# Attention stage of a fused attention and mixing kernel: three engines' loops written out, waits against constants, covered waits left out

## The chip, the cores and the metric

The kernel runs on one core of a Trainium2 chip. The metric is the device time of one execution in microseconds (us). Before the change three runs took 1269.08, 1270.90 and 1271.06 us, median 1270.9.

## What is computed

Inputs are q, k, v of shape (8, 8, 576, 64), batch, heads, sequence, head dimension, in float32, and the weights of two mixing layers.

```python
scores = scale * np.matmul(q, k.transpose(0, 1, 3, 2))
thresh = np.max(scores, axis=-1, keepdims=True) - tau
scores = np.where(scores >= thresh, scores, -1000000000.0)
attn = np.exp(scores - np.max(scores, axis=-1, keepdims=True))
attn = attn / (np.sum(attn, axis=-1, keepdims=True) + 1e-09)
x = np.matmul(attn, v)                  # then heads side by side: (8, 576, 512)
...
xk, xr = mu_k * x + (1 - mu_k) * x_prev, mu_r * x + (1 - mu_r) * x_prev
x = sigmoid(xr @ w_r) * (np.maximum(xk @ w_k, 0.0) ** 2 @ w_v)
gate = sigmoid(causal convolution of x with 5 taps)
out = (gate * (x @ w_val)) @ w_out
```

## The kernel before

Each engine has its own program, and the programs meet in semaphores alone: an instruction raises a count when it is done, and a wait holds an engine until a count is reached. The kernel has two stages. The attention stage takes the 64 heads in 32 pairs. The mixing stage takes the sequence in 16 halves and isn't touched; TensorE's program for it is already written out.

In the attention stage a pair of heads (2 x 576 queries) makes nine score tiles of 128 queries by 576 keys: tiles 0 to 7 alternate between the heads, tile 8 (MIX) holds the last 64 queries of both. For each tile TensorE makes the scores into one of three PSUM slots (`score_ps`, L606; four matmuls of 288 columns, six for tile 8), VectorE takes the row maximum (`max`, L791), ScalarE the exponential (`exp`, L717), and VectorE multiplies it with the mask of the threshold and sums the row (`mask`, L803, followed by a read of the accumulator, which raises `probs_ready`). A `thr` step (L797) makes the thresholds of two tiles at a time. Then TensorE transposes the tile's four blocks (`probs`, L549) into one of two further PSUM banks (`aux_ps`), ScalarE copies the bank out (L697) and raises `aux_copied`, and after all tiles TensorE multiplies with v (`pv0`, `pv1`, L651). The remainders go the same way (`rem0`, `rem1`). The next pair's q and k are transposed by TensorE (`k0`, `q0`, and `kq0`, one block of both remainders), copied by ScalarE, split into a high and a low part by GpSimd, and stacked below one another by DMA from SyncE's queue.

The order on each engine is written out by hand in a plan, and a step with a minus belongs to the pair before:

```python
PE_PLAN = steps("""
    scores1 kq0 scores3 k0 pv0- scores2 probs4- scores4 q0 rem1- scores0 probs5- scores8 probs1
    probs7- scores6 probs6- probs8- scores7 probs3 pv1- rem0 scores5 probs0 probs2
""")
DVE_PLAN = steps("""
    max1 max3 thr4- mask5- thr0 sum0- mask1 mask3 max2 recip0- max4 thr1 mask2 max0 mask4 max8 thr2
    mask0 max6 max7 thr3 mask8 mask6 mask7 max5
""")
```

The number is that of the tile, not of the turn. A score step waits in `probs_ready` for the mask of the tile three turns earlier, which had its slot: scores8 for the mask of tile 2, scores7 for that of tile 0. Steps that write a bank of `aux_ps` wait in `aux_copied` for the copy two groups earlier: kq0 for the copy of probs0.

`walk` (L329) runs the plans: the first pair, then a hardware loop of 15 rounds with two pairs each (pairs 1 to 30), then the last pair without k, q and kq, and a drain. In the loop, the count that a wait needs depends on the round, so it is computed in a register by `count`, `count_later`, `turns`; in the first pair, the last and the drain the round is the number 0 and the counts are constants. GpSimd's and SyncE's programs of this stage have loops of their own. At the end of the stage the drain overlaps with the mixing stage's first matmuls.

Of the kernel before, what the change touches and what calls it, by code (L numbers as in the profile page):

```python
# [14 lines left out]
TILES = 9  # L15
MIX = 8
# [99 lines left out]
def attention(nc, banks, semaphore, q, k, v, tau, small_loads, x_first, weights, x_scratch, recip_scratch, w_hi, w_lo,  # L116
# [18 lines left out]
    with ExitStack() as ctx:  # L135
# [409 lines left out]
        def tensor(pe):  # L545
# [21 lines left out]

            def run(plan, it, c):
                for kind, i, before in plan:
                    cc = c - 1 if before else c  # L570
                    if kind in GROUPS:
                        g = number(c, (kind, i, before))
                        if g >= 2:
                            pe.wait_ge(aux_copied, turns(it, g - 1))
                        bank = aux_ps[g % 2]
                        blocks = bank[:].rearrange("p (t q) -> p t q", t=4)
                    if kind == "scores":
                        par = cc % 2
                        if SCORE_TURN[i] == 0:
                            if cc > 0:  # L580
                                pe.wait_ge(q_stacked[par], count_later(it, cc, 2))
                                pe.wait_ge(k_stacked[par], count_later(it, cc, 2))
                        if cc == 0:

                            pe.wait_ge(first_lo, 4 if i < MIX and i % 2 else 8)

                        turn = SCORE_TURN[i]
                        if turn >= SLOTS:
                            pe.wait_ge(probs_ready, count(it, cc, TILES, MASK_TURN[BY_TURN[turn - SLOTS]] + 1))
                        elif cc > 0:  # L590
                            pe.wait_ge(probs_ready, count(it, cc - 1, TILES, MASK_TURN[BY_TURN[turn - SLOTS]] + 1))
# [17 lines left out]
                    elif kind == "probs":  # L609
                        pe.wait_ge(probs_ready, count(it, cc, TILES, MASK_TURN[i] + 1))  # L610
# [3 lines left out]
                    elif kind == "rem":  # L614

                        pe.wait_ge(probs_ready, count(it, cc, TILES, 1 + max(
# [4 lines left out]
                        if i == 1:  # L621
                            transpose_mixed(blocks[:, 2, :], probs[:, MIX, MAIN:S])
                            pe.wait_ge(recip_ready, count(it, cc, 1, 1))
                            last = transpose(blocks[0:TILES, 3, :], recip[:])
                    elif kind == "k":
                        if c == 0:

                            pe.wait_ge(first_lo, 6)
                        pe.wait_ge(k_loaded[(c + 1) % 2], count_later(it, c + 1, 3))
                        for t in range(FULL):  # L630
                            last = transpose(blocks[:, t, :], qk_nat[:, (c + 1) % 2, 1, t, :])
                    elif kind == "q":
                        pe.wait_ge(q_loaded[(c + 1) % 2], count_later(it, c + 1, 3))
                        for t in range(FULL):
                            last = transpose(blocks[:, t, :], qk_nat[:, (c + 1) % 2, 0, t, :])
                    elif kind == "kq":
                        pe.wait_ge(k_loaded[(c + 1) % 2], count_later(it, c + 1, 3))
                        pe.wait_ge(q_loaded[(c + 1) % 2], count_later(it, c + 1, 3))
                        last = transpose(blocks[:, 0, :], rem_nat[:, (c + 1) % 2, :])
                    elif kind == "pv":  # L640
                        needed = [("probs", n) for n in ((0, 1, 2, 3), (4, 5, 6, 7, 8))[i]] + [("rem", i)]
                        n = max(number_of(cc, *x) for x in needed) if c == PAIRS else number_of(cc, *latest(needed))
                        pe.wait_ge(aux_copied, turns(it, 1 + n))
                        if i == 0:
                            pe.wait_ge(v_loaded[cc % 2], count_loaded(it, cc, 3))
                        cols = slice(QA, S) if i else slice(0, QA)
                        for t in range(FULL + 1):
                            for h in range(2):
                                m = probsT[:, t, h, cols] if t < FULL else probsT_rem[:, cols]
                                values = v_nat[:, cc % 2, h * FULL + t, :] if t < FULL else v_rem[:, cc % 2, h, :]  # L650
                                last = nc.tensor.matmul(bank[D * h:D * (h + 1), 0:cols.stop - cols.start],  # L651
                                                        values, m, start=(t == 0), stop=(t == FULL))
                    elif kind == "hidden":

                        pe.wait_ge(probs_ready, count(it, PAIRS - 1, TILES, MASK_TURN[BY_TURN[6 + i // 2]] + 1))
                        pe.wait_ge(w_split, 2 * UNITS + 2)
                        ahead.hidden(pe, i)
# [34 lines left out]
            walk(run, pe, PE_FIRST, PE_PLAN, PE_DRAIN)  # L692
            pe.wait_ge(aux_copied, len(FIRST_RUN) + (PAIRS - 2) * PER_PAIR + len(LAST_RUN) + len(DRAIN_RUN))

        def scalar(act):
# [6 lines left out]

            def run(plan, it, c):
                for kind, i, before in plan:
                    cc = c - 1 if before else c
                    if kind in GROUPS:
                        g = number(c, (kind, i, before)) if (kind, i, before) in FULL_RUN else number_of(cc, kind, i)
                        act.wait_ge(aux_full, turns(it, g + 1))
                        bank = aux_ps[g % 2]
                        blocks = bank[:].rearrange("p (t q) -> p t q", t=4)  # L710
                    if kind in ("k", "kq") and c > 0:

                        act.wait_ge(own_steps, count(it, c - 1, 3, 3))
                    if kind == "exp":
                        act.wait_ge(max_ready, count(it, cc, TILES, MAX_TURN[i] + 1))
# [25 lines left out]
                    elif kind == "pv":  # L741
                        if i == 0:

                            act.wait_ge(x_ready, count(it, cc, 1, 1))
# [22 lines left out]
            walk(run, act, ACT_FIRST, ACT_PLAN, ACT_DRAIN, ACT_EXTRA)  # L767

        def vector(dve):
# [14 lines left out]

            def run(plan, it, c):
                for kind, i, before in plan:
                    cc = c - 1 if before else c
                    if kind == "max":
                        dve.wait_ge(scores_full, count(it, cc, TILES, SCORE_TURN[i] + 1))
# [3 lines left out]
                    elif kind == "thr":  # L793
                        turns_of = THRESHOLDS[i]
                        group = slice(turns_of.start, turns_of.stop)
                        dve.wait_ge(max_ready, count(it, cc, TILES, turns_of.stop))
                        nc.vector.tensor_reduce(threshold[:, group], neg_max[:, group, :], mybir.AxisListType.X, ALU.add,  # L797
                                                negate=True).then_inc(threshold_ready, 1)
                    elif kind == "mask":
                        turn = MAX_TURN[i]  # L800
                        dve.wait_ge(threshold_ready, count(it, cc, len(THRESHOLDS), turn // 2 + 1))
                        dve.wait_ge(exp_done, count(it, cc, TILES, EXP_TURN[i] + 1))
# [6 lines left out]
                    elif kind == "sum":  # L809
                        dve.wait_ge(probs_ready, count(it, cc, TILES, TILES))  # L810
                        nc.vector.tensor_reduce(divisor[:], row_sum[:, cc % 2, :, :], mybir.AxisListType.X,
                                                ALU.add).then_inc(sum_ready, 1)
                    elif kind == "recip":
                        dve.wait_ge(sum_ready, count(it, cc, 1, 1))
# [29 lines left out]
            walk(run, dve, DVE_FIRST, DVE_PLAN, DVE_DRAIN, DVE_EXTRA)  # L844
# [607 lines left out]
```

## Time and profile before

| | us |
|---|---|
| median of three runs | 1270.9 |
| the profiled execution | 1269.48 |
| its span, first to last instruction | 1267.4 |
| TensorE matmuls busy | 1256.4 (99%) |
| VectorE busy | 921.6 (73%) |
| ScalarE busy | 782.1 (62%) |
| GpSimd busy | 421.2 (33%) |

The attention stage fills about the first 548 us, the mixing stage the rest. PE is TensorE's matmuls, PEld its weight loads, which overlap with matmuls, PEldq the sequencer of TensorE; DVE is VectorE, ACT ScalarE, POOL GpSimd, SP SyncE. Register, branch and semaphore instructions aren't counted as busy. A line number such as L549 can be that of a helper (transposes) that many steps use.

### The profile page before, as it was taken

The page shows a single profiled execution, that of the slowest core. Times are in us where ns is not written, and L with a number is a line of the kernel's source. Part 1 is how long each engine was busy: PE and PEld are TensorE (multiplying, and loading weights), DVE is VectorE, ACT ScalarE, POOL GpSimd, SP SyncE. Part 2 cuts the span into 40 slices and gives each one's busy share as a digit, 9 for nine tenths or more (in the row PEclk, how much of TensorE's full clock was granted, in tenths as well). Part 3 has the DMA queues.
Part 4 walks back from the last instruction along what each step waited for, and adds up shares of the span by engine and source line. Part 5 has one row for each costly group of instructions (what it writes and reads, how often), then busy time and mean ns, then how long its engine had stood idle before and what let it go on. Part 6 is the DMA issues. An engine that isn't in the chain of part 4 may idle for free.

```text
span 1267.4 us, 29655 instructions
## 1 busy us (share of the span) xinstructions
PE 1256.4 (99%) x9347; PEld 1129.0 (89%) x9347; DVE 921.6 (73%) x2159; ACT 782.1 (62%) x1729; POOL 421.2 (33%) x498
## 2 busy tenths in 40 slices
PE   7999999999999999999999999999999999999999
PEld 6887788777788788789999999999999999999998
DVE  6888888888888888868657657665756666476644
ACT  5888888888888888865455445445534544444432
POOL 4687877777787876452000000000000000000000
PEclk9999999999999999999999999999999999999999
DMA  5566656666666665421110110111011011001001
GB/s 124 142 160 156 164 151 160 167 165 159 167 160 156 165 166 141 108 74 36 37 33 4 36 45 3 36 37 37 1 45 37 1 36 37 27 19 37 18 1 42
DMA packets 136344, 104.17 MB, mean 82 GB/s; under 512 B 91328, under 2 KB 107968, under 8 KB 136256
## 3 DMA queue, kind: packets, MB, share of 16 engines
q1 hardware_dynamic: 134912, 102.78, 30.6%
q8 instruction: 45, 0.74, 0.2%
q10 hardware_dynamic: 1344, 0.30, 0.1%
q14 instruction: 43, 0.35, 0.1%
HBM read 54.56 MB, written 19.02 MB: 58 GB/s over the span
## 4 chain that ended last, share of the span: by engine, by line
PE 98%; DVE 1%; ACT 0%; issue 0%; POOL 0%; POOLq 0%
PE score_ps L1090 32%; PE score_ps L1177 16%; PE aux_ps L549 14%; PE score_ps L606 14%; PE aux_ps L651 13%; PE aux_ps L1161 8%; PE aux_ps L564 1%; DVE neg_max L791 0%; DVE probs L803 0%; PE score_ps L665 0%; PE score_ps L671 0%; DVE q_all L826 0%; ACT probsT L697 0%; ACT probs L717 0%; DVE k_all L819 0%
## 5 line engine op out<-in xcount | busy, mean ns | idle before, releaser
L791 DVE TENSOR_REDUCE neg_max<-score_ps 128x1 f32<-128x576 f32 x288 | 217.4, 755 | 57.6 <-PE score_ps L606 52.4
L803 DVE SCALAR_TENSOR_TENSOR probs<-score_ps,threshold,probs 128x576 f32<-128x576 f32 x288 | 230.3, 817 | 7.5 <-ACT probs L717 0.5
L1090 PE MATMUL score_ps<-xm_hi,w_hi 128*128 128x288 f32 x768 | 226.5, 295 | 0.0
L1090 PE MATMUL score_ps<-xm_lo,w_hi 128*128 128x288 f32 x768 | 226.4, 295 | 0.0
L1090 PE MATMUL score_ps<-xm_hi,w_lo 128*128 128x288 f32 x768 | 225.7, 294 | 0.0
L717 ACT ACTIVATE probs<-score_ps,neg_max 128x576 f32<-128x576 f32 x288 | 206.5, 743 | 4.8 <-DVE neg_max L791 4.5
L606 PE MATMUL score_ps<-k_all,q_all 128*128 128x288 f32 x1032 | 201.3, 317 | 4.9 <-DVE probs L803 4.9
L697 ACT ACTIVATE probsT<-aux_ps 128x512 f32<-128x512 f32 x288 | 161.6, 595 | 51.9 <-PE aux_ps L549 50.8
L549 PE MATMUL aux_ps<-ident,probs 128*128 128x128 f32 x1280 | 184.8, 275 | 0.5 <-ACT probsT L697 0.5
L1082 POOL MEMSET x_in<- 128x4 f32 x7 | 0.7, 105 | 519.8 <-DVE mixed L1219 519.8
L549 PEld LDWEIGHTS aux_ps<-ident,probs 128*128 128x128 f32 x1280 | 149.7, 140 | 18.0 <-issue 15.1
L606 PEld LDWEIGHTS score_ps<-k_all,q_all 128*128 128x128 f32 x1032 | 146.0, 190 | 18.7 <-issue 17.6
L1177 PE MATMUL score_ps<-kk_hi,w_hi 128*128 128x288 f32 x512 | 151.1, 295 | 0.0
L1177 PE MATMUL score_ps<-kk_lo,w_hi 128*128 128x288 f32 x512 | 150.9, 295 | 0.0
L1177 PE MATMUL score_ps<-kk_hi,w_lo 128*128 128x288 f32 x512 | 150.2, 293 | 0.0
L1359 DVE SCALAR_TENSOR_TENSOR gate<-x,taps,gate 128x288 f32<-128x288 f32 x256 | 132.1, 516 | 18.7 <-ACT gate L1257 15.3
L1090 PEld LDWEIGHTS score_ps<-xm_hi,w_lo 128*128 128x128 f32 x768 | 144.4, 188 | 0.5 <-issue 0.5
L1090 PEld LDWEIGHTS score_ps<-xm_hi,w_hi 128*128 128x128 f32 x768 | 144.4, 188 | 0.0
L1090 PEld LDWEIGHTS score_ps<-xm_lo,w_hi 128*128 128x128 f32 x768 | 144.3, 188 | 0.0
L651 PE MATMUL aux_ps<-probsT,v_nat 128*64 128x320 f32 (+1 forms) x1024 | 138.3, 412 | 0.0
L651 PEld LDWEIGHTS aux_ps<-probsT,v_nat 128*64 128x64 f32 x1024 | 67.8, 136 | 48.7 <-issue 10.6
L1304 DVE TENSOR_TENSOR square<-relu 128x288 f32<-128x288 f32 x128 | 57.2, 457 | 69.2 <-ACT relu L1247 64.0
(106 smaller groups left out, 2460.2 us busy)
## 6 DMA issues: line engine op xcount, KB each, us to landing
k_all<-k_all SPq DMA_DIRECT2D x31, 320.0 KB, 4.4
q_all<-q_lo SPq DMA_DIRECT2D x62, 160.0 KB, 4.2
recip_rows<-recip_scratch SPq DMA_DIRECT2D x64, 144.0 KB, 3.5
x_scratch<-x_out SPq DMA_DIRECT2D x32, 288.0 KB, 2.2
out<-y SPq DMA_DIRECT2D x36, 256.0 KB, 2.1
k_all<-k_all SPq DMA_DIRECT2D x31, 288.0 KB, 3.5
v_nat<-in_v SPq DMA_DIRECT2D x32, 256.0 KB, 2.8
qk_nat<-in_q SPq DMA_DIRECT2D x63, 128.0 KB, 2.6
```

Source lines behind the costliest of these rows:

```text
L549: return nc.tensor.transpose(out, in_, ident[:])
L606: last = nc.tensor.matmul(ps[:, half, 0:HALF], q_part, k_part, start=(n == 0), stop=(n == len(terms) - 1))
L651: last = nc.tensor.matmul(bank[D * h:D * (h + 1), 0:cols.stop - cols.start], values, m, start=(t == 0), stop=(t == FULL))
L697: return nc.scalar.activation(out, in_, ACT.Copy)
L717: nc.scalar.activation(tile_halves(i), scored(i), ACT.Exp, bias=neg_max[:, turn, 0:1], scale=1.0).then_inc(exp_done, 1)
L791: nc.vector.tensor_reduce(neg_max[:, turn, 0:1], scored(i), mybir.AxisListType.XY, ALU.max, negate=True).then_inc(max_ready, 1)
L803: nc.vector.scalar_tensor_tensor(tile_halves(i), scored(i), threshold[:, turn:turn + 1], tile_halves(i), ALU.is_ge, ALU.mult, accum_out=ro ...
L1090: last = nc.tensor.matmul(ps, w, m, start=(n == 0), stop=(n == 3 * len(terms) - 1))
L1161: last = nc.tensor.matmul(y_ps[i % 2][:], g[:, ch, col:col + P], w[:, ch, :], start=(n == 0), stop=(n == 3 * C - 1))
L1177: last = nc.tensor.matmul(kv_ps[u][:, 0:HT], w, m[:, j, :], start=(n == 0), stop=(n == 3 * CF - 1))
L1304: nc.vector.tensor_tensor(square[:, i % 4, :], relu[:, i % 2, :], relu[:, i % 2, :], ALU.mult).then_inc(square_done, 1)
L1359: nc.vector.scalar_tensor_tensor(gate[:, u, :], x2[:, u, t:t + HT], taps[:, t, u:u + 1], gate[:, u, :], ALU.mult, ALU.add).then_inc(conv_s ...
```

## The change

TensorE, ScalarE and VectorE no longer loop in the attention stage: `walk_out` emits all 32 pairs one after the other with the round 0, so that every count is a constant. Their waits go through `once`, which keeps the highest count that this engine has waited for on each semaphore and emits a wait only if its count is higher. A `pv` step makes one wait on `aux_copied` where it made two. The order of the steps, all computing instructions and their operands, and the programs of GpSimd and SyncE stay as they are. Cut to its core (all further waits of the three engines are replaced in the same way):

```diff
-        def walk(run, eng, start, plan, drain, extra={}):
+        def once(eng):
+            reached = {}
+            def wait(signal, value):
+                if reached.get(signal, 0) < value:
+                    reached[signal] = value
+                    eng.wait_ge(signal, value)
+            return wait
+        def walk_out(run, start, plan, drain, extra={}):
             run(start, 0, 0)
-            with eng.Fori(0, (PAIRS - 2) // 2) as it:
-                run(plan, it, 1)
-                run(plan, it, 2)
+            for c in range(1, PAIRS - 1):
+                run(plan, 0, c)
             run(last(plan, extra), 0, PAIRS - 1)
             run(drain, 0, PAIRS)
...
+            wait = once(pe)
             def run(plan, it, c):
...
                         g = number(c, (kind, i, before))
-                        if g >= 2:
-                            pe.wait_ge(aux_copied, turns(it, g - 1))
+                        if g >= 2 and kind != "pv":
+                            wait(aux_copied, turns(it, g - 1))
...
                         if turn >= SLOTS:
-                            pe.wait_ge(probs_ready, count(it, cc, TILES, MASK_TURN[BY_TURN[turn - SLOTS]] + 1))
+                            wait(probs_ready, count(it, cc, TILES, MASK_TURN[BY_TURN[turn - SLOTS]] + 1))
...
                         if i == MIX and cc > 0:
-                            pe.wait_ge(own_steps, count(it, cc - 1, 3, 3))
+                            wait(own_steps, count(it, cc - 1, 3, 3))
...
                     elif kind == "probs":
-                        pe.wait_ge(probs_ready, count(it, cc, TILES, MASK_TURN[i] + 1))
+                        wait(probs_ready, count(it, cc, TILES, MASK_TURN[i] + 1))
...
                     elif kind == "kq":
-                        pe.wait_ge(k_loaded[(c + 1) % 2], count_later(it, c + 1, 3))
-                        pe.wait_ge(q_loaded[(c + 1) % 2], count_later(it, c + 1, 3))
+                        wait(k_loaded[(c + 1) % 2], count_later(it, c + 1, 3))
+                        wait(q_loaded[(c + 1) % 2], count_later(it, c + 1, 3))
...
-                        pe.wait_ge(aux_copied, turns(it, 1 + n))
+                        wait(aux_copied, turns(it, max(1 + n, g - 1)))
...
-            walk(run, pe, PE_FIRST, PE_PLAN, PE_DRAIN)
+            walk_out(run, PE_FIRST, PE_PLAN, PE_DRAIN)
...
-            walk(run, act, ACT_FIRST, ACT_PLAN, ACT_DRAIN, ACT_EXTRA)
+            walk_out(run, ACT_FIRST, ACT_PLAN, ACT_DRAIN, ACT_EXTRA)
...
                     elif kind == "mask":
                         turn = MAX_TURN[i]
-                        dve.wait_ge(threshold_ready, count(it, cc, len(THRESHOLDS), turn // 2 + 1))
-                        dve.wait_ge(exp_done, count(it, cc, TILES, EXP_TURN[i] + 1))
+                        wait(threshold_ready, count(it, cc, len(THRESHOLDS), turn // 2 + 1))
+                        wait(exp_done, count(it, cc, TILES, EXP_TURN[i] + 1))
...
-            walk(run, dve, DVE_FIRST, DVE_PLAN, DVE_DRAIN, DVE_EXTRA)
+            walk_out(run, DVE_FIRST, DVE_PLAN, DVE_DRAIN, DVE_EXTRA)
```

## Rows read from the trace of the kernel before

**Rows 1.** The page: a line on the chain, one of the costliest groups.
```profile
PE 98%; DVE 1%; ACT 0%; issue 0%; POOL 0%; POOLq 0%
...
L549 PE MATMUL aux_ps<-ident,probs 128*128 128x128 f32 x1280 | 184.8, 275 | 0.5 <-ACT probsT L697 0.5
```

**Rows 2.** Busy time by stretches: stretch, length, PE, PEld, DVE, ACT, POOL, clock, DMA share, GB/s.
```profile
122.00:300.00 178.00, 178.00 (x1403) 141.82 (x1402) 154.30 (x361) 143.81 (x287) 139.67 (x160) 1.00 0.64 163
...
600.00:900.00 300.00, 300.00 (x2134) 292.21 (x2133) 192.09 (x456) 146.47 (x369) 0.31 (x3) 1.00 0.09 28
```

**Rows 3.** The chain in order of time: start, length, what; both are pv1.
```profile
38.78 2.84 PE aux_ps L651 x20
...
524.19 2.84 PE aux_ps L651 x20
```

**Rows 4.** Timeline of TensorE's matmuls: start, length, engine, line, operation, count.
```profile
232.13 0.60 PE L549 MATMUL aux_ps<-ident,probs 128*128 128x128 f32 x4
232.49 0.78 PE L606 MATMUL score_ps<-k_all,q_all 128*128 128x288 f32 x4
...
238.41 0.77 PE L606 MATMUL score_ps<-k_all,q_all 128*128 128x288 f32 x4
239.02 0.60 PE L549 MATMUL aux_ps<-ident,probs 128*128 128x128 f32 x4
...
243.98 0.77 PE L606 MATMUL score_ps<-k_all,q_all 128*128 128x288 f32 x4
...
245.40 0.60 PE L549 MATMUL aux_ps<-ident,qk_nat 128*128 128x128 f32 x4
```

**Rows 5.** Timeline of ScalarE and the loads at kq0; L637 on TensorE's sequencer.
```profile
243.83 0.60 ACT L697 ACTIVATE probsT<-aux_ps 128x512 f32<-128x512 f32 x1 [0.58 <-PE aux_ps L549]
...
244.63 0.14 PEld L549 LDWEIGHTS aux_ps<-ident,rem_nat 128*128 128x128 f32 x1
...
L637 PEldq ALU_OP  x1: 32/32/32, 244.5 to 244.5; - x1
```

**Rows 6.** Timeline of ScalarE and the loads in the drain.
```profile
544.48 0.60 ACT L697 ACTIVATE probsT<-aux_ps 128x512 f32<-128x512 f32 x1 [0.58 <-PE aux_ps L549]
...
545.12 0.20 PEld L549 LDWEIGHTS aux_ps<-ident,probs 128*128 128x128 f32 x2 [0.49 <-ACT probsT L697]
```

**Rows 7.** Timelines of VectorE, ScalarE and the loads, scores8 to scores7.
```profile
235.03 0.75 DVE L791 TENSOR_REDUCE neg_max<-score_ps 128x1 f32<-128x576 f32 x1
235.75 0.82 DVE L803 SCALAR_TENSOR_TENSOR probs<-score_ps,threshold,probs 128x576 f32<-128x576 f32 x1
...
238.21 0.08 DVE L803 DVE_READ_ACCUMULATOR probs<-score_ps,threshold,probs 128x1 f32 x1
...
234.93 0.71 ACT L717 ACTIVATE probs<-score_ps,neg_max 128x576 f32<-128x576 f32 x1
...
235.24 0.19 PEld L606 LDWEIGHTS score_ps<-k_own,q_own 128*128 128x128 f32 x1
...
238.38 0.19 PEld L606 LDWEIGHTS score_ps<-k_all,q_all 128*128 128x128 f32 x1
...
254.94 0.09 DVE L803 DVE_READ_ACCUMULATOR probs<-score_ps,threshold,probs 128x1 f32 x1
...
255.08 0.19 PEld L606 LDWEIGHTS score_ps<-k_all,q_all 128*128 128x128 f32 x1
```

**Rows 8.** Instruction queues, 62 to 530 us, then 600 to 900 (packets, MB, share); a wait.
```profile
q14 instruction: 4, 0.03, 0.0%
...
q8 instruction: 17, 0.28, 0.4%
...
DVE square L1304 <- issue: 5.2, 2, 2.6
```

**Rows 9.** Issues on SyncE's queue; the page's row on them (count, KB, us to landing).
```profile
238.59 1.27 SPq L327 DMA_DIRECT2D q_all<-q_lo  x1
...
q_all<-q_lo SPq DMA_DIRECT2D x62, 160.0 KB, 4.2
```

More of the change, by code:

```diff
@@ L614, in run @@
                     elif kind == "rem":
-                        pe.wait_ge(probs_ready, count(it, cc, TILES, 1 + max(
+                        wait(probs_ready, count(it, cc, TILES, 1 + max(
                             MASK_TURN[n] for n in (range(FULL) if i == 0 else range(FULL, TILES)))))
@@ L622, in run @@
                             transpose_mixed(blocks[:, 2, :], probs[:, MIX, MAIN:S])
-                            pe.wait_ge(recip_ready, count(it, cc, 1, 1))
+                            wait(recip_ready, count(it, cc, 1, 1))
                             last = transpose(blocks[0:TILES, 3, :], recip[:])
@@ L653, in run @@
                     elif kind == "hidden":
[L655 to L656 removed]
+                        wait(probs_ready, count(it, PAIRS - 1, TILES, MASK_TURN[BY_TURN[6 + i // 2]] + 1))
+                        wait(w_split, 2 * UNITS + 2)
                         ahead.hidden(pe, i)
@@ L701, in scale_q @@
                 return nc.scalar.activation(out, in_, ACT.Copy, scale=q_scale[:, 0:1])
+            wait = once(act)
             def run(plan, it, c):
@@ L711, in run @@
                     if kind in ("k", "kq") and c > 0:
-                        act.wait_ge(own_steps, count(it, c - 1, 3, 3))
+                        wait(own_steps, count(it, c - 1, 3, 3))
                     if kind == "exp":
-                        act.wait_ge(max_ready, count(it, cc, TILES, MAX_TURN[i] + 1))
+                        wait(max_ready, count(it, cc, TILES, MAX_TURN[i] + 1))
                         turn = MAX_TURN[i]
@@ L742, in run @@
                         if i == 0:
-                            act.wait_ge(x_ready, count(it, cc, 1, 1))
+                            wait(x_ready, count(it, cc, 1, 1))
                         cols = slice(QA, S) if i else slice(0, QA)
@@ L783, in vector @@
             nc.vector.memset(row_sum[:, :, :, 1], 1e-9).then_inc(tau_steps, 1)
+            wait = once(dve)
             def run(plan, it, c):
@@ L788, in run @@
                     if kind == "max":
-                        dve.wait_ge(scores_full, count(it, cc, TILES, SCORE_TURN[i] + 1))
+                        wait(scores_full, count(it, cc, TILES, SCORE_TURN[i] + 1))
                         turn = MAX_TURN[i]
@@ L795, in run @@
                         group = slice(turns_of.start, turns_of.stop)
-                        dve.wait_ge(max_ready, count(it, cc, TILES, turns_of.stop))
+                        wait(max_ready, count(it, cc, TILES, turns_of.stop))
                         nc.vector.tensor_reduce(threshold[:, group], neg_max[:, group, :], mybir.AxisListType.X, ALU.add,
@@ L809, in run @@
                     elif kind == "sum":
-                        dve.wait_ge(probs_ready, count(it, cc, TILES, TILES))
+                        wait(probs_ready, count(it, cc, TILES, TILES))
                         nc.vector.tensor_reduce(divisor[:], row_sum[:, cc % 2, :, :], mybir.AxisListType.X,
@@ L813, in run @@
                     elif kind == "recip":
-                        dve.wait_ge(sum_ready, count(it, cc, 1, 1))
+                        wait(sum_ready, count(it, cc, 1, 1))
                         nc.vector.reciprocal(recip[:], divisor[:]).then_inc(recip_ready, 1)
```

18 lines of the change are left out of this document (9 added, 9 removed).

## Prediction

> **What bounds the kernel now.** I read the page's chain first: what ended last is 98% TensorE [rows 1]. Matmul ends are modelled, so this names the engine but doesn't show how much of its time is stalls. The table by stretches says the clock was 1.00 (the level of 2.4 GHz) in the attention loop as in the mixing stage, so clock is no part of the question [rows 2]. The chain of waits gives the loop's period: from the second head's value product (pv1) of the second pair at 38.78 us to that of the last looped pair at 524.19 are 29 pairs, 16.74 us each [rows 3]. That is 502 of 1269.48 us (30 looped pairs). The change can only shorten this period; the mixing stage is the same code.
>
> Then I go through the timeline of one pair and ask which of TensorE's steps take longer than the same step elsewhere. That is where waits and register operations can be on the path; where matmuls follow one another at their usual distance, they aren't.
>
> **Part 1, the one-block transpose kq0.** A score tile of four matmuls takes 0.61 us until the next step starts (238.41 to 239.02). Four transposes show 0.60, of which the last takes 0.27 by the page's mean, so they start (0.60 - 0.27) / 3 = 0.11 apart; ahead of a score tile four take 0.36 (232.13 to 232.49), a single one 0.36 - 3 x 0.11 = 0.03 [rows 1, 4]. scores1, kq0, scores3 should take 0.61 + 0.03 + 0.61 = 1.25 us. They take 243.98 to 245.40 = 1.42 [rows 4]. The loss is 0.17 per pair. Why: kq0 waits for the copy out of its bank. That copy ended at 243.83 + 0.60 = 244.43, but kq0's load started at 244.63, 0.20 later. Between them, at 244.5, TensorE's sequencer ran L637's computation of a count for the k wait, and by the code L638's wait for q follows it [rows 5]. By the order of the code the copy's wait comes before both, so nothing of kq0 was in the queue when the copy ended, and each costs its whole time. In the drain, where counts are constants already, the load starts 0.04 to 0.05 us after such a copy (544.48 + 0.60 = 545.08, load 545.12) [rows 6]. With the change kq0 has no computation left. Its k and q loads were there long before, so those waits cost nothing as long as they are passed before the copy ends; then the copy's wait is the last, as in the drain. It could start at 244.48. Unheld it would start when the last score matmul does, 244.63 - 0.17 = 244.46, so nothing of the 0.17 is left. Gain 0.17 x 30 = 5.1 us, which is also the upper end; the lower is 0 (rival B). Less than 0 is excluded, as no wait is added to the step.
>
> **Part 2, scores8 and what is late next.** scores8 waits for VectorE's mask of tile 2, whose accumulator read starts with the next max at 235.03 and takes 0.08; the load started at 235.24, 0.13 after its end. L594, a count for own_steps, stands between. The direct distance is 0.05 (254.94 + 0.09 = 255.03 to the load of scores7 at 255.08), so 0.08 could go [rows 7]. But I don't add it. What is late next is scores7, which waits for the mask of tile 0: accumulator read ended 238.21 + 0.08 = 238.29, load 238.38, 0.09 later; in the next pair it is the 0.05 just named, so that pair is bound there already [rows 7]. By the timeline VectorE works from max4 to that mask with hardly a gap. One gap is the change's to take. mask4 starts 0.72 after max0 started (235.03 to 235.75), where max0's 0.75 less the overlap of 0.07 to 0.08 by which the next one starts before its end (as the read and max0 at 235.03 do) gives 0.68; its exp ended at 234.93 + 0.71 = 235.64 [rows 7]. It has two waits, and the one for the threshold is covered by mask2's, so the exp wait moves onto the instruction and about 0.04 goes. The stretch from scores4 to scores7 thus gains 0.04 in one pair of two, and in the other 0.04 plus the 0.03 of slack (0.09 less 0.06): 0.05 on average, 1.5 us in 30 pairs. Ends: 0, and 0.08 for scores8 with as much again for steps held in the same way that I don't cost, 0 to 5 us.
>
> **Part 3, answers of nothing.** All other dropped waits and register operations of TensorE lie beside queued matmuls: 0. ScalarE's too: the copies and exps follow one another or wait for TensorE. If VectorE or ScalarE's cover goes, scores7 shows it first. First pair, last pair and drain have constants before: under 0.3 us.
>
> **Part 4, what it adds.** Code. 30 pairs of some 146 loads and as many matmuls, some 9,000 instructions, come from memory once instead of from a loop. Between 62 and 530 us no block came on the queue q8 (only 4 on q14, the other engines'); in the mixing stage, written out for TensorE already, 17 came in 300 us, with TensorE busy 300.00 of 300.00 [rows 2, 8]. At 2134 matmuls (so 4268 instructions) for 17 blocks, a block holds about 250; the loop would need some 36, one in 13 us. The attention stage has its DMA engines busy 0.64 against 0.09, so a block may queue longer, but 13 us is far over the 4.2 us that even the stacking of q takes to land [rows 2, 9]. Cost 0; bounds 0 and VectorE's price of 2.6 us for a missed block, 36 x 2.6 = 94 us [rows 8]. A block could also push back the stacking of q: second issue 238.59, landing 4.2 later at 242.8, scores1 at 243.98, slack 1.2 us [rows 4, 9]. That hides it.
>
> A rule of the Trainium skill bears on this (Runtime: NRT & Kernel Launch, Instruction fetch mechanics): sequential fetch is mostly hidden, a taken branch out of the window stalls, so written-out code is preferred. By it the loop's 15 back edges would give something besides. This trace agrees on the first half: 17 blocks in a stretch without an idle TensorE [rows 2, 8]. On the second no block came on q8 from 62 to 530 us, so no edge fetched one. Another (Advanced Engine Details and Errata, Sequencer Loop) speaks against the change: the sequencer reads ahead while engine instructions wait in a queue. By it alone the register work would be worth nothing; [rows 5] show the place where the queue was empty.
>
> **Sum.** 5.1 + 1.5 = 6.6 us: 1269.48 - 6.6 = 1262.9 for a run like the profiled one, which lies 1.4 under the median of three (1270.9; 1269.08 to 1271.06). From the median: 1264.3 us, -0.52%.
>
> **Rivals.**
> A, the forecast: 1264.3, chance 0.62.
> B, the held steps are bound by what they wait for, not by the operations between. If kq0's load stays 0.2 after its copy (three waits, whose order the compiler chooses, so that the copy wait blocks the sequencer again), only part 2 remains: 1270.9 - 1.5 = 1269.4. Against it stand the drain's 0.05 [rows 6]. Chance 0.11, within 0.2%. Here belongs also that the written-out program isn't different where it matters.
> C, VectorE doesn't hold scores7, because its chain starts earlier too: part 1 and scores8 in full and as much again for other held steps, 0.17 + 0.16 = 0.33 x 30 = 10: 1270.9 - 10 = 1261. Against it the 0.05 of the second pair [rows 7]. Chance 0.13.
> D, another wait eats half (ScalarE's copy for kq0 gets late once scores1 comes earlier): 1267.5. Chance 0.09, most of it still faster by over 0.2%.
> E, the other side: blocks of code arrive late amid the stacking traffic. Each late block stalls TensorE; from 6.6 / 36 = 0.18 us a block the gain is gone, from 0.25 us the kernel is slower by over 0.2%; at 0.5 us it is 1270.9 - 6.6 + 18 = 1282. For it: DMA share 0.64, and a stall of 2.6 us twice on VectorE in the mixing stage, where it loops [rows 8]. Against: 13 us of notice. Chance 0.05.
>
> **How the numbers follow.** This kernel's runs differ by 0.15%, so about 0.2% (2.5 us) can be told from no change. Faster: A 0.62 + C 0.13 + most of D 0.08 = 0.83 and a little of B, 0.84. Slower: 0.05. Same: 0.11. The range of 8 in 10 takes in A with 1.5 us of spread between runs, C, and D: 1260.5 to 1268.3; it leaves out E, B and the far end of C.
>
> **What would show it.** After the change the chain should have pv1 rows about 16.52 us apart; kq0's load within 0.06 of its copy and scores1 to k0 1.25 us; scores8's load 0.06 behind the accumulator read and every scores7 at 0.05 to 0.06; no ALU rows under L637, L594 and their like on the three engines; some 36 more instruction packets on q8, no new idle of the loads at equal steps of 250 instructions. The mixing stage should be as long as before. The forecast is wrong if the period stays above 16.65 or scores7 isn't the held step, and wrong in sign if TensorE idles every 13 us or scores1 waits for a stack.

## The result, and the profile after

The changed kernel took 1277.38 us in the median (1276.45 to 1280.75, 6 runs), the kernel before, run beside it, 1269.74 (1268.89 to 1271.06). The ratio is 1.0065, 95% interval 1.0053 to 1.0077: slower by some 8 us where 1264.3 was forecast. The profiled execution is the slowest of the six, 1280.75 us with a span of 1278.9; before it was 1269.48 and 1267.4.

The page of the changed kernel: the instruction queues, the chain by engine, and TensorE's score matmuls with the idle time ahead of them.

```profile
q8 instruction: 74, 1.21, 0.4%
q14 instruction: 57, 0.47, 0.1%
...
PE 77%; SPq 12%; DMA 5%; issue 3%; DVE 1%; ACT 1%; POOL 1%; POOLq 0%
...
L620 PE MATMUL score_ps<-k_all,q_all 128*128 128x288 f32 x1032 | 198.2, 318 | 15.8 <-DMA q_all<-q_lo 10.9
```

Before, TensorE held 98% of the chain [rows 1]. Now it holds 77%. Most of the rest, 17%, is SyncE's queue and the transfers that it issues. The score matmuls stand idle for the stacking of q, which none did before. The waits of the whole run (engine, line, waited for, us in total, times, longest) say how often:

```profile
PE score_ps L620 <- DMA q_all<-q_lo: 10.9, 11, 2.0
...
DVE square L1323 <- issue: 9.5, 2, 4.8
```

By stretches (columns as in [rows 2]), TensorE is idle in the attention stage for 4.0 us of 178 and 7.1 of 180. Before, the first of these had no idle time [rows 2]. The mixing stage has only 0.46 in 300.

```profile
122.00:300.00 178.00, 173.99 (x1377) 139.12 (x1375) 148.35 (x353) 141.23 (x283) 135.69 (x156) 1.00 0.63 161
300.00:480.00 180.00, 172.89 (x1363) 138.72 (x1358) 147.50 (x353) 139.20 (x278) 137.86 (x157) 0.99 0.62 158
600.00:900.00 300.00, 299.54 (x2127) 291.43 (x2126) 191.99 (x458) 148.51 (x375) 0.32 (x3) 1.00 0.09 28
```

**The undisturbed pairs are what was forecast.** The chain's value products, the first of two successive pairs and then that of the last looped pair:

```profile
45.60 2.31 PE aux_ps L666 x20
62.07 2.31 PE aux_ps L666 x20
...
523.79 2.31 PE aux_ps L666 x20
```

The first two are 16.47 us apart, as the next ones are, where 16.52 was forecast and 16.74 was the period before [rows 3]. But from 45.60 to 523.79 there are 28 pairs, so the mean is 17.08. From kq0 to kq0, 13 of 29 pairs stay within 0.1 us of 16.5, and the rest take up to 18.8. The long ones lie between 176 and 333 us and between 382 and 490.

**What the long pairs wait for.** SyncE's queue in two of them (start, length, what; x2 is two issues in one row):

```profile
421.17 1.41 SPq L290 DMA_DIRECT2D qk_nat<-in_q  x2
422.76 1.69 SPq L296 DMA_DIRECT2D rem_nat<-in_q  x1
...
437.85 0.37 SPq L372 DMA_DIRECT2D x_scratch<-x_out  x1
438.47 2.71 SPq L290 DMA_DIRECT2D qk_nat<-in_q  x2
441.37 0.62 SPq L296 DMA_DIRECT2D rem_nat<-in_q  x1
```

The issue of rem_nat<-in_q took 1.69 us at 422.76 and 0.62 at 441.37. The pair of qk_nat issues took 1.41 at 421.17 and 2.71 at 438.47. It is the same instruction each time. What was different is seen in the queues of four short windows, 422.4 to 424.5, 424.5 to 426.6, 438.9 to 441.2 and 441.2 to 443.3 us (packets, MB, share). A block of TensorE's code, one 16 KB packet on q8, came in the first and the third, none in the second and the fourth:

```profile
q1 hardware_dynamic: 1007, 0.25, 53.6%
q8 instruction: 1, 0.02, 4.5%
...
q1 hardware_dynamic: 681, 0.17, 35.7%
...
q1 hardware_dynamic: 605, 0.34, 50.7%
q8 instruction: 1, 0.02, 5.0%
...
q1 hardware_dynamic: 709, 0.19, 38.2%
```

Between 62 and 530 us 29 blocks came on q8 in the changed kernel, against none before [rows 8]. Of SyncE's issues between 25 and 560 us, 14 took 0.35 us or more over the median of their kind, 0.35 to 1.34 each and 10.7 in all. Thirteen of them overlap the fetch of a block on q8, and the fourteenth ends 0.1 us before one begins. A fifteenth has no other of its kind in the trace: x_in<-x_scratch took 1.89 us at 456.29, during a block, and 0.57 in the kernel before. Most overlaps lengthen no issue by that much, though: of the 508 issues of the frequent kinds between 62 and 530 us, 40 overlap a block's fetch, and 12 of these were stretched; of the other 468 one was.

The chain between them (start, length, what) shows why a longer issue holds TensorE:

```profile
430.41 4.22 DMA q_all<-q_lo
...
434.68 0.80 PE score_ps L620 x4
...
437.35 0.33 POOL x_out L523
```

There is a ring. SyncE stores x_out, then issues the loads of the next q and k, the stores of the reciprocals, the stacks of k and q, and recip_rows. GpSimd makes x_out from recip_rows behind that, and SyncE waits for x_out before the next round. scores1 waits for the stack of q. The chain reaches GpSimd by way of scores1, because the profile puts GpSimd's wait down to the semaphore update nearest before it. By the code GpSimd waits there for recip_rows, for the copy of an earlier value product and for the last store, and in all 27 rounds between 62 and 530 us the next store starts 1.99 to 2.02 us after recip_rows has landed (2.00 to 2.03 in the kernel before). So the ring is closed by recip_rows, without TensorE, and TensorE hangs on it by scores1. From store to store (L372, 419.96 and 437.85) are 17.89 us: 12.41 to the last issue of recip_rows, 1.07 of them the stretched issue, 3.48 to its landing, and 2.00 to the store.

**Not every long pair has a stretched issue.** Between 98 and 258 us there is none, and yet the pairs from 176 to 262 us take 16.8 to 17.7. The trace shows two other delays in the ring. The first is a late landing of recip_rows (start, length, what), whose median is 3.5 us on the page of the kernel before:

```profile
240.59 4.88 DMA recip_rows<-recip_scratch
```

In the changed kernel four rounds have 4.2 to 5.1 us, 4.7 us over the usual in all, and three of the four overlap a block's fetch. In the twelve traces of this case together, between 62 and 530 us, recip_rows took over 4.1 us in 26 of the 38 rounds in which a block was fetched meanwhile, and in 3 of the 295 others.

The second has nothing to do with blocks. In four of its rounds SyncE issues two small loads for the mixing stage between the store and the next loads of q and k. Those loads come 1.98 to 3.30 us after the store there, and 0.62 to 1.20 us after it in the other rounds. The four pairs concerned take 17.17, 17.46, 17.80 and, where a block was fetched during the second load, 18.81 us:

```profile
456.29 1.89 SPq L439 DMA_DIRECT2D x_in<-x_scratch  x1
```

The small loads are in the kernel before too, where no pair is over 16.83 us.

The theory, called **F** in what was expected of the runs: blocks of TensorE's code stretch SyncE's issues and transfers, and the ring of SyncE, DMA and GpSimd has nearly no slack against TensorE's pace. The main rival, **R**: a faster TensorE upsets the ring by itself, and the blocks merely come along.

### The profile page after: what moved, and what is told of

Read it like the earlier page. It is cut to its first block, busy times and chain, and to the rows that moved or that the text cites. A ratio compares the mean times of both kernels' runs of the same rounds, so it can differ in the third digit from the quotient of the medians.

```text
span 1278.9 us, 26925 instructions
## 1 busy us (share of the span) xinstructions
PE 1256.0 (98%) x9347; PEld 1129.9 (88%) x9347; DVE 914.8 (72%) x2159; ACT 781.3 (61%) x1729; POOL 421.2 (33%) x498
## 4 chain that ended last, share of the span: by engine, by line
PE 77%; SPq 12%; DMA 5%; issue 3%; DVE 1%; ACT 1%; POOL 1%; POOLq 0%
PE score_ps L1109 32%; PE score_ps L1196 16%; PE aux_ps L1180 8%; PE aux_ps L561 7%; PE score_ps L620 7%; PE aux_ps L666 6%; SPq L290 3%; DMA recip_rows<-recip_scratch 3%; DMA q_all<-q_lo 2%; SPq L296 2%; SPq L326 1%; SPq L356 1%; SPq L378 1%; SPq L355 1%; SPq L327 1%
## 5 line engine op out<-in xcount | busy, mean ns | idle before, releaser
L810 DVE TENSOR_REDUCE neg_max<-score_ps 128x1 f32<-128x576 f32 x288 | 214.8, 755 | 76.2 <-PE score_ps L620 70.9
L620 PE MATMUL score_ps<-k_all,q_all 128*128 128x288 f32 x1032 | 198.2, 318 | 15.8 <-DMA q_all<-q_lo 10.9
L1378 DVE SCALAR_TENSOR_TENSOR gate<-x,taps,gate 128x288 f32<-128x288 f32 x256 | 132.3, 517 | 18.7 <-ACT gate L1276 15.3
L666 PEld LDWEIGHTS aux_ps<-probsT,v_nat 128*64 128x64 f32 x1024 | 68.1, 137 | 49.2 <-issue 11.1
```

The costliest lines, as they stand in the source:

```text
L620: last = nc.tensor.matmul(ps[:, half, 0:HALF], q_part, k_part, start=(n == 0), stop=(n == len(terms) - 1))
L810: nc.vector.tensor_reduce(neg_max[:, turn, 0:1], scored(i), mybir.AxisListType.XY, ALU.max, negate=True).then_inc(max_ready, 1)
L1378: nc.vector.scalar_tensor_tensor(gate[:, u, :], x2[:, u, t:t + HT], taps[:, t, u:u + 1], gate[:, u, :], ALU.mult, ALU.add).then_inc(conv_s ...
```

## The experiments

**1. TensorE faster, no blocks.** The kernel before with its loops. Only the order of two waits is changed, which gives most of part 1 and 2 without writing anything out.

```diff
-                        if g >= 2:
+                        if g >= 2 and kind != "kq":
                             pe.wait_ge(aux_copied, turns(it, g - 1))
...
                         pe.wait_ge(q_loaded[(c + 1) % 2], count_later(it, c + 1, 3))
+                        if g >= 2:
+                            pe.wait_ge(aux_copied, turns(it, g - 1))
```

The wait for own_steps moves in the same way ahead of the one for probs_ready at scores8.

> The kernel before with its loops, but TensorE gets part of the gain without any written-out code: at kq0 the wait for the copy comes after the waits for k and q, and at scores8 the wait for the mask comes after that for own_steps, so that the wait satisfied last stands on the weight load. Theory F (instruction blocks fetched for TensorE's written-out program hold up SyncE's issues and the transfers of a ring of SyncE, DMA and GpSimd that has nearly no slack): no blocks are fetched in the loop, TensorE's pair drops from 16.74 to about 16.5 to 16.6 us, the ring holds, and the time is 1263 to 1266 us. Rival R (the ring alone can't follow a faster TensorE, blocks or not): the time doesn't fall, 1269 to 1278 us, with waits of score loads for the stacking of q.

It took 1264.81 us (1264.44 to 1266.45), ratio 0.9965 (0.9951 to 0.9980). Pairs take 16.54 to 16.58 us, with three exceptions of 17.02 to 17.14. The first two of these are rounds with the small loads. The chain by engine, the q8 row of 62 to 530 us, and the wait for q's stack:

```profile
PE 88%; SPq 6%; DMA 2%; issue 2%; DVE 1%; POOL 0%; ACT 0%; POOLq 0%
...
q8 instruction: 1, 0.02, 0.0%
...
PE score_ps L606 <- DMA q_all<-q_lo: 0.8, 3, 0.3
```

TensorE's pace is nearly that of the changed kernel's good pairs, and the ring holds it for 0.8 us in all instead of 10.9. So pace alone isn't the cause. It isn't free either: SyncE is on 6% of the chain. No run has the full pace of 16.47 us without blocks.

**2. TensorE slower again, with the blocks.** The changed kernel with kq0's transpose issued three times, so that a pair takes as long as before.

```diff
-                        last = transpose(blocks[:, 0, :], rem_nat[:, (c + 1) % 2, :])
+                        for _ in range(3):
+                            last = transpose(blocks[:, 0, :], rem_nat[:, (c + 1) % 2, :])
```

> The changed kernel with kq0's transpose issued three times instead of once (same result), which adds 2 x 0.11 us of TensorE to a pair: unheld its pair would take 16.47 + 0.22 = 16.69 us, as long as before the change, while its blocks are fetched as before. Theory F: the fetches alone make the ring too slow, the time stays near the changed kernel's, 1274 to 1280 us. Rival R (only the faster TensorE upsets the ring): the time returns to that of before, 1268 to 1271 us.

1282.23 us (1279.09 to 1287.14), ratio 1.0090 (1.0072 to 1.0108), above even the 1280 that F named. Undisturbed pairs take 16.69 to 16.71 us, just under those before, and still others take 17 to 18.8. The wait for q's stack, and a landing on the chain:

```profile
PE score_ps L620 <- DMA q_all<-q_lo: 10.9, 9, 1.9
...
212.46 5.23 DMA recip_rows<-recip_scratch
```

With the pace of before and the blocks of after, the wait is as long as in the changed kernel (10.9 us). R falls. At this pace the ring has more room than in the changed kernel, 0.37 us a pair (16.70 less 16.33, the mean of two rounds in experiment 1), and the loss is larger still. That isn't due to the stretched issues (11, 6.3 us in all) but to late landings: recip_rows took 4.15 to 5.23 us in 11 rounds, 13.4 us over the usual together, and in ten of the 11 a block was fetched meanwhile.

**3. ScalarE and VectorE alone written out,** TensorE's program as before.

> Only ScalarE's and VectorE's programs are written out; TensorE's keeps its loop and its waits. Theory F with TensorE's blocks as the cause: their blocks are few (under 20 of 8 KB in the stage), TensorE stays at 16.7 us a pair, and the time is 1267 to 1270.5 us. If any written-out program does the harm: 1273 us or more.

1270.56 us (1269.34 to 1272.08, 10 runs), at the upper end of the range named, ratio 1.0006 (0.9996 to 1.0015), pairs 16.65 to 16.8 us. Their code comes on q14, and 19 blocks between 62 and 530 us left the pairs alone. No issue of SyncE's there was stretched by over 0.2 us in that stretch. These blocks are half as large (57 packets, 0.47 MB on the page, so 8 KB each, against 16 KB on q8).

**4. TensorE alone written out,** ScalarE and VectorE looping as before.

> TensorE's program alone is written out, with constants and covered waits left out; ScalarE and VectorE keep their loops. Theory F (TensorE's blocks of code hold up the ring of SyncE's issues, transfers and GpSimd's steps, which has no slack) takes the whole loss to come from TensorE's blocks: about as slow as the changed kernel in the attention stage, some 28 blocks on q8 between 62 and 530 us, pairs of 16.5 to 18.5 us, 1275 to 1279 us in all, with VectorE's first square in the mixing stage at 2.6 us as in the kernel before instead of 4.8. Rival V (part of the loss comes from VectorE's and ScalarE's written-out programs: their blocks on q14 and what they fetch at the stage's border): 1270 to 1273 us, with longer pairs rarer than in the changed kernel.

1274.90 us (1272.73 to 1276.51), ratio 1.0038 (1.0024 to 1.0051). That lies between the two ranges that were named, at the edge of F's. The q8 row of 62 to 530 us, and two waits:

```profile
q8 instruction: 29, 0.48, 0.4%
...
PE score_ps L629 <- DMA q_all<-q_lo: 6.7, 9, 1.5
...
DVE square L1332 <- issue: 5.2, 2, 2.6
```

Long pairs of 17 to 18.3 us are back, with ten of SyncE's issues stretched by 0.35 us or more between 62 and 530 us. Undisturbed pairs take 16.54 us, the pace of experiment 1, which has no blocks, and the medians lie 10.1 us apart. So TensorE's code gives the larger part, 0.38 of 0.65%. The loss isn't the sum of 3 and 4 (0.06 + 0.38 = 0.44%). Of what is missing, VectorE's stalls behind the attention stage make 1.5 us; how the remainder splits wasn't measured.

**5 and 6. Both cases in one kernel.** Experiment 1's kernel, with TensorE's pairs written out in one half only. Here every wait is kept, which also tests whether the left-out waits matter. Below is the first of the two, with its numbers put in; it holds for TensorE alone, and ScalarE and VectorE keep their loops. The mirror writes out pairs 1 to 16 and loops from 8 to 15.

```diff
-            with eng.Fori(0, (PAIRS - 2) // 2) as it:
+            with eng.Fori(0, 7) as it:
                 run(plan, it, 1)
                 run(plan, it, 2)
+            for c in range(15, 31):
+                run(plan, 0, c)
```

> The loop with the swapped waits (1264.8 us) for pairs 1 to 14; from pair 15 on TensorE's program alone is written out, with every wait kept. So one kernel holds both cases at the same pace. Theory F: pairs of 16.54 us with no block of TensorE's code up to about 257 us, then some 15 blocks and held pairs of 17 to 18.5 us after it, and none before; 1266 to 1273 us. If written-out TensorE code held no ring, or if the held pairs of the changed kernel come from the waits that it leaves out (here all are kept), pairs stay at 16.54 us: 1264 to 1266 us. If the held pairs come of the place in the run (191 to 333 us in the changed kernel) and not of the blocks, those from 191 to 257 us are long too.

1272.04 us (1270.07 to 1274.35), ratio 1.0018 (1.0008 to 1.0028). Busy times of 90 to 257 us, then 257 to 330 and 330 to 520:

```profile
90.00:257.00 167.00, 167.00 (x1335) 135.04 (x1332) 145.27 (x343) 136.41 (x272) 133.23 (x151) 1.00 0.64 163
...
257.00:330.00 73.00, 71.38 (x569) 57.09 (x566) 61.83 (x147) 58.40 (x117) 55.48 (x64) 1.00 0.62 159
...
330.00:520.00 190.00, 185.30 (x1470) 149.20 (x1469) 161.05 (x379) 150.97 (x300) 141.91 (x162) 1.00 0.61 155
```

> The mirror: pairs 1 to 16 of TensorE's program written out with every wait kept, pairs 17 to 30 in the loop with the swapped waits. Theory F: blocks and held pairs up to about 290 us alone, and from there on pairs of 16.54 us, with at most two or three of 17.0 as the swapped loop had; 1266 to 1273 us. If a ring that was once upset stays upset, pairs over 17.2 us go on behind 300 us. Without an effect of blocks: 1264 to 1266 us.

1271.99 us (1268.3 to 1274.6), ratio 1.0012 (1.0000 to 1.0023). The first and the last of the same stretches:

```profile
90.00:257.00 167.00, 163.57 (x1296) 131.91 (x1295) 141.54 (x334) 133.20 (x265) 129.16 (x146) 1.00 0.61 157
...
330.00:520.00 190.00, 188.32 (x1499) 151.48 (x1498) 163.98 (x387) 153.64 (x306) 143.01 (x164) 1.00 0.64 161
```

In the second-half kernel no block came from 90 to 257 us, TensorE is never idle there, and every pair takes 16.53 to 16.58 us. With the 17 blocks from 257 to 520 us come 6.3 us of idle time and pairs of up to 18.7. In the mirror, 11 blocks and 3.4 us idle lie in the first stretch. Three long pairs follow from 280 to 333 us, with the last four blocks (277.8 to 322.4). From there to 520 us no block comes, and nine of the eleven pairs are within 0.05 us of 16.55; the two others take 17.01 and 16.81, and both are rounds with the small loads, like two of the three exceptions of experiment 1. From 179 to 230 us the mirror has three pairs of 17.0 to 17.4, and the second-half kernel none. So the place in the run isn't the cause, and the ring recovers within a pair or so when the blocks stop. All waits were kept, so leaving them out isn't needed for the loss.

**7. The ring's slack.** The changed kernel with one step of SyncE moved. It no longer waits for x_out at the end of its round, but behind the loads of the next one.

```diff
                     load_k(sp, it, c + 2)
+                if c > 1:
+                    store_x(it, c - 2)
...
                 if c == PAIRS:
                     ahead.next_x(sp)
-                if c > 0:
                     store_x(it, c - 1)
```

> The changed kernel, but SyncE stores a pair's x only after it has issued the q and k loads of the next round, so it no longer waits for recip_rows to land and for GpSimd's multiplication before those loads. That takes some 5 us of waiting out of its ring and leaves all fetches in place. If the ring's lack of slack is what turns a held issue into time (part of both theories): pairs of 16.47 us throughout, 1262 to 1264 us. If the blocks stall TensorE itself, or the mixing stage takes the loss: 1270 us or more.

1264.42 us (1263.6 to 1266.03), ratio 0.9956 (0.9939 to 0.9972): 13 us less than the changed kernel, and 0.4 over the range named. The q8 row, an issue (its usual length for this pair is 1.23), and the wait for q's stack:

```profile
q8 instruction: 30, 0.49, 0.4%
...
428.72 2.08 SPq L290 DMA_DIRECT2D qk_nat<-in_k  x2
...
PE score_ps L621 <- DMA q_all<-q_lo: 2.0, 2, 1.7
```

The blocks come as before, and 14 issues are still stretched by 0.35 us or more, 11.7 together. But 27 of 29 pairs take 16.46 to 16.66 us. One of the two others, 18.4 us long, has an issue of v_rem that took 2.08 us as a block came, and the other, of 17.05, is a round with the small loads. So the stretched issues don't cost by themselves, only where the ring has no room.

**8. Control for the move:** the same move in the kernel before.

> Control for the moved store: the kernel before, with its loops, and SyncE's store_x moved behind the next round's q and k loads. If the ring sets no pace in the kernel before (TensorE's 16.74 us a pair are longer than the ring's 16.1), nothing changes: 1269 to 1271 us, pairs of 16.7 us. If the move is worth something by itself, whatever the blocks do, 1262 to 1266 us, and the gain of the changed kernel with the moved store says nothing of the blocks.

1269.83 us (1268.57 to 1271.05, 10 runs), ratio 1.0000 (0.9990 to 1.0009), pairs 16.70 to 16.80 us. The move is worth nothing without blocks at this pace, and 0.2 us at 16.55 us a pair (experiment 10). The 13 us of experiment 7 come with the blocks.

**9. TensorE alone written out, store moved.**

> TensorE alone written out, and the store moved. By theory F the blocks still lengthen SyncE's issues but the ring has room for them, and VectorE keeps its loop and its short stall of 2.6 us at the border of the stages: 1262 to 1265 us, 1 to 2 us less than the changed kernel with the moved store (1264.4). If VectorE's written-out program gave part of the gain in the pairs (mask4's wait), pairs are 0.04 us longer than there: 1264 to 1266 us.

1263.83 us (1263.32 to 1264.12), ratio 0.9951 (0.9936 to 0.9967). It is the lowest median of all and 11.1 us under experiment 4, which differs in the moved store alone. All but two of its pairs (16.66 and 17.04) take 16.53 to 16.56 us instead of 16.47, as was expected if VectorE's written-out program gives a part of the gain. The time is even 0.2 us under the 1264 to 1266 named for that case, and VectorE's short stall at the border of the stages goes with it.

**10. Loops, swapped waits, store moved.**

> Loops kept, the two waits of TensorE swapped, and SyncE's store_x moved. By theory F the loop with the swapped waits had a few pairs of 17.0 us because its period had come within 0.4 us of the ring's; with the store out of the ring these go, 16.5 us in all pairs: 1262 to 1264 us, faster than the kernel before, the changed kernel and the swapped loop (1264.8). If those few pairs had another cause (transfers that collide, not the issues of the ring), it stays at 1264 to 1266 us.

1264.64 us (1263.45 to 1265.0), ratio 0.9957 (0.9943 to 0.9970). All pairs take 16.53 to 16.58 us and the exceptions of experiment 1 are gone, as expected. The median, though, is only 0.17 us under that of experiment 1, where three long pairs of 0.5 us each had been there to gain, and it lies just outside the expected range. Whether most runs of experiment 1 have fewer long pairs than its profiled one isn't known. Experiments 1, 7, 9 and 10 all beat both kernels, and their intervals overlap. The simplest of them is experiment 1: two waits swapped, nothing written out.

## Why the prediction was wrong

**Part 1 (kq0, 5.1 us) and part 2 (1.5 us): right in mechanism, and nearly in size.** TensorE's scores1, scores3 and k0 in the changed kernel, the steps of [rows 4] (kq0 lies between the first two, at 143.32):

```profile
142.71 0.77 PE L620 MATMUL score_ps<-k_all,q_all 128*128 128x288 f32 x4
143.35 0.77 PE L620 MATMUL score_ps<-k_all,q_all 128*128 128x288 f32 x4
143.96 0.60 PE L561 MATMUL aux_ps<-ident,qk_nat 128*128 128x128 f32 x4
```

142.71 to 143.96 are 1.25 us, the forecast to the hundredth. scores8's and scores7's loads, the accumulator reads that they wait for, and mask4 between them:

```profile
133.82 0.08 DVE L822 DVE_READ_ACCUMULATOR probs<-score_ps,threshold,probs 128x1 f32 x1
133.96 0.82 PEld L620 LDWEIGHTS score_ps<-k_own,q_own 128*128 128x128 f32 x6
...
134.49 0.81 DVE L822 SCALAR_TENSOR_TENSOR probs<-score_ps,threshold,probs 128x576 f32<-128x576 f32 x1
...
136.95 0.08 DVE L822 DVE_READ_ACCUMULATOR probs<-score_ps,threshold,probs 128x1 f32 x1
137.09 0.56 PEld L620 LDWEIGHTS score_ps<-k_all,q_all 128*128 128x128 f32 x4
```

Both loads start 0.06 behind the read, as foretold, where scores8's was 0.13 before [rows 7]. mask4 starts 0.67 us after max0 (133.82), where it was 0.72 [rows 7]: part 2's 0.04, and a hundredth more. An undisturbed pair takes 16.47 us, 0.05 less than the sum said. With VectorE and ScalarE looping it takes 16.54 to 16.55 (experiments 4 and 9), so their written-out programs give 0.08 a pair where part 2 said 0.05. Rivals B and D fall. C's mechanism falls, since scores7 still waits for its mask; in size the gain of 0.27 us a pair lies midway between A's 0.22 and C's 0.33. The gain is real in every kernel in which the ring has room.

**Part 3** wasn't refuted: experiments 5 and 6 keep all waits and have good pairs of 16.55 us, and so does experiment 9, in which TensorE's covered waits are left out.

**Part 4 failed, and with it the sum.** Its words were "Cost 0" for the blocks and, for the stacking of q, "slack 1.2 us [...] That hides it". Three things in this step were wrong.

First, it looked at one slack, from the landing of q's stack to scores1. What precedes the stack is SyncE's round, which it didn't follow. That round was to be read in the trace before. SyncE's queue there, two rounds:

```profile
407.91 1.18 SPq L375 DMA_DIRECT2D recip_rows<-recip_scratch  x2
...
424.74 1.16 SPq L375 DMA_DIRECT2D recip_rows<-recip_scratch  x2
...
440.84 1.17 SPq L375 DMA_DIRECT2D recip_rows<-recip_scratch  x2
```

The round from 424.74 to 440.84 takes 16.10 us and the one before it 16.83, against TensorE's 16.74. SyncE's loop has two rounds, and in one of them more time passes between the store and the next load. How long both take when little holds them is seen in experiment 1, store by store:

```profile
326.94 0.38 SPq L360 DMA_DIRECT2D x_scratch<-x_out  x1
...
343.05 0.37 SPq L360 DMA_DIRECT2D x_scratch<-x_out  x1
...
359.59 0.38 SPq L360 DMA_DIRECT2D x_scratch<-x_out  x1
```

16.11 and 16.54 us, 32.65 together, against 32.94 for two of TensorE's new pairs. That is 0.15 us of slack a pair, where a stretched issue takes 0.35 to 1.34 more and a late recip_rows 0.8 to 1.7. The 16.1 that the expectation of experiment 8 names for the ring is its shorter round alone. The four rounds with the small loads take 17.5 to 18.2 us in experiment 1, so they use up what slack there is even without blocks.

Second, a block was priced by what it may do to TensorE, a stall for lack of code, by VectorE's 2.6 us. In the attention stage TensorE didn't stall for code: none of its matmuls' idle time there is put down to issue, the name that VectorE's stalls have. Its idle time is that of the waits shown above, and what a block cost was on SyncE's issues and on the transfer of recip_rows. The number of blocks was too high as well: 29 more than before came on q8 (74 against 45), not some 36.

Third, "what is late next" was asked of VectorE and scores7 only. Next was SyncE.

**Rival E had the sign and not the mechanism.** It foretold 1282 us at 0.5 us a block, from TensorE stalls, and had 0.05 of the chance. The measured loss against the forecast, 1277.4 - 1264.3 = 13.1 us over 29 blocks, is 0.45 a block, but in unequal parts: the blocks of the first 176 us cost next to nothing, later pairs lose 0.3 to 2.3 us each, and a part of that is the small loads'. The list of signs did name the right one, "scores1 waits for a stack". Its argument against, 13 us of notice, holds for the code's arrival and says nothing about who shares the way. The rule on sequential fetch (the Trainium skill, Runtime: NRT & Kernel Launch, Instruction fetch mechanics) was taken as support. TensorE's own fetch was indeed hidden, as the rule says. The runs show the cost beside it.

**The mixing stage** wasn't "as long as before": VectorE's two stalls there grew from 2.6 us [rows 8] to 4.8. The last kq0 comes 10.0 us later than before (522.56 against 512.53) and the span is 11.5 longer (1278.9 - 1267.4), so 1.5 us are lost behind it, and the stalls are the one difference found there. The other traces agree: from the last kq0 to the end of the span are 754.8 to 754.9 us in the eight kernels in which VectorE loops and 756.3 to 757.3 in the four in which it is written out.

## What to carry to other kernels

Before writing a looped engine program out, follow the round of each DMA-issuing queue from one issue to the same issue a round later, and compare it with the period that the change is to bring. Take every kind of round, those with a load that comes once too: here the shorter round showed 0.37 us of room, both kinds together 0.15, and four rounds none. Look first for the cheap part of the gain: here the order of two waits, with the one that is satisfied last placed last, gave most of it without a byte of code. A wait that a queue can pass later (the store behind the next loads) is worth nothing until something else in its round grows, and then it was worth 11 to 13 us.

## What the hardware showed that was not expected

An issue on SyncE's queue can take longer while a 16 KB block of TensorE's code is fetched: rem_nat<-in_q 1.69 us instead of 0.63, a pair of qk_nat issues 2.71 instead of 1.41. The 8 KB blocks of the other engines did not show this (19 of them in experiment 3 and no stretched issue). In all twelve traces between 62 and 530 us, 75 of the 268 issues that overlap a 16 KB block's fetch were stretched by 0.35 us or more, and 2 of some 5,900 others. The transfer of recip_rows takes longer too, up to 5.2 us instead of 3.5. SyncE's next loads are issued during that transfer in rounds without a block as well, where it kept its 3.5 in nearly all, so they alone aren't the cause. Why issue and transfer are longer, whether by the DMA engines or by the descriptors' way, wasn't separated, nor why only one overlap in four or so stretches an issue.

VectorE's first square after the edge of its mixing loop stalls for longer when VectorE's attention program is written out. In experiment 7, start, length, what and the idle time before it:

```profile
767.07 0.83 DVE L1324 TENSOR_TENSOR square<-relu 128x288 f32<-128x288 f32 x2 [5.23 <-issue]
```

The longest was 4.8 to 5.4 us in every kernel in which VectorE is written out (the changed kernel, experiments 2, 3 and 7), and 2.6 to 2.9 in every one in which it loops (experiments 1, 4, 5, 6, 8, 9, 10 and the kernel before). The stall comes some 200 us after the code that was changed. The traces show one fetch more in it: before, two blocks on q14 start at 767.5 and 767.6 and the stall ends at 769.66; in the changed kernel two start at 777.7 and 777.8, a third at 780.1, and it ends at 781.85. So VectorE waits for two fetches one behind the other. That the target of the jump lies differently in its block now is a guess; no run tried it.
